# Block-local attention: one resident copy of the value bands, their block sums taken from it, keys in quarters, the score scale moved into the mask addition

## What is computed

```python
k_sum = k.reshape(B, H, nb, block, D).max(axis=3)
v_sum = v.reshape(B, H, nb, block, D).mean(axis=3)
scores_l = scale * np.matmul(q, k.transpose(0, 1, 3, 2))      # kept where |i - j| < 16
scores_s = scale * np.einsum('bhsd,bhnd->bhsn', q, k_sum) + np.log(block)
a = softmax(np.concatenate([scores_l_m, scores_s], axis=-1))
out = np.matmul(a, np.concatenate([v, v_sum], axis=2))
```

## Time and profile before

| | us |
|---|---|
| median of 3 runs (lowest, highest) | 466.71 (465.79, 468.4) |
| the profiled execution, by itself | 468.67 |
| its span, first to last instruction | 466.6 |
| PE busy, share of the span | 427.0, 92% |
| DVE, ACT, POOL busy | 242.4, 188.7, 55.3 |

### The profile page before, as it was taken

The page is one execution under the profiler, slowest core; times in us unless marked ns, Lnnn a source line. Parts: engine busy times, 40 slices in busy tenths (PEclk is TensorE's granted clock), DMA queues, the critical chain, the costliest instruction groups (busy, mean ns, idle before and its releaser), DMA issues.

```text
span 466.6 us, 8147 instructions
## 1 busy us (share of the span) xinstructions
PE 427.0 (92%) x2811; PEld 341.2 (73%) x2812; DVE 242.4 (52%) x381; ACT 188.7 (40%) x425; POOL 55.3 (12%) x96
## 2 busy tenths in 40 slices
PE   8589887298999999999999897999999899999997
PEld 3478776156888888888888654888887688888775
DVE  4678895676226362244511316666666745546252
ACT  1857895702336363363522423333333331222010
POOL 3223421111100010000200054000000000000000
PEclk9978999779999999999999899999999999999999
DMA  8988792845911118211103056000000000000012
GB/s 330 317 265 284 274 340 89 323 150 173 396 63 46 45 45 346 81 45 45 46 22 112 25 155 228 1 0 1 1 0 1 0 24 22 22 24 21 26 45 91
DMA packets 12909, 52.77 MB, mean 113 GB/s; under 512 B 1744, under 2 KB 1872, under 8 KB 11344
## 3 DMA queue, kind: packets, MB, share of 16 engines
q1 hardware_dynamic: 7584, 37.44, 21.8%
q0 software_dynamic: 3424, 11.54, 7.7%
q10 hardware_dynamic: 1872, 3.41, 1.9%
HBM read 61.82 MB, written 11.53 MB: 157 GB/s over the span
## 4 chain that ended last, share of the span: by engine, by line
PE 74%; DVE 12%; ACT 5%; DMA 4%; issue 2%; POOL 0%; DVEq 0%; SPq 0%; ACTq 0%; POOLq 0%
PE ps L1107 14%; PE ps L1109 14%; PE ps L1108 14%; PE ps L1220 6%; PE ps L1222 6%; PE ps L1221 6%; PE ps L1010 2%; PE ps L1185 2%; PE ps L1135 2%; ACT p L527 2%; DMA v<-v_win 2%; PE ps L1114 2%; DMA kfull<-k_full 1%; PE ps L985 1%; PE ps L995 1%
## 5 line engine op out<-in xcount | busy, mean ns | idle before, releaser
L1220 PE MATMUL ps<-z_h,mix_h 128*128 128x512 f32 x144 | 56.9, 395 | 0.9 <-DVE z_l L944 0.9
L1222 PE MATMUL ps<-z_h,mix_l 128*128 128x512 f32 x144 | 56.2, 390 | 0.0
L1221 PE MATMUL ps<-z_l,mix_h 128*128 128x512 f32 x144 | 56.1, 390 | 0.0
L1107 PE MATMUL ps<-w_h,hT_h 128*128 128x512 f32 x104 | 42.3, 407 | 1.9 <-DVE hT_l L856 1.9
L1107 PE MATMUL ps<-w_h,xT_h 128*128 128x512 f32 x104 | 41.6, 400 | 1.9 <-DVE xT_l L850 1.9
L1109 PE MATMUL ps<-w_l,hT_h 128*128 128x512 f32 x104 | 41.4, 398 | 0.0
L1108 PE MATMUL ps<-w_h,hT_l 128*128 128x512 f32 x104 | 41.2, 397 | 0.0
L527 ACT ACTIVATE p<-s,bias 128x120 f32<-128x120 f32 x96 | 36.5, 383 | 11.7 <-DVE bias L707 11.5
L856 DVE TENSOR_TENSOR hT_l<-ps,hT_h 128x512 fp32r<-128x512 f32 x26 | 16.7, 685 | 46.3 <-ACT hT_h L594 46.3
L1109 PE MATMUL ps<-w_l,xT_h 128*128 128x512 f32 x104 | 40.6, 390 | 0.0
L1108 PE MATMUL ps<-w_h,xT_l 128*128 128x512 f32 x104 | 40.6, 390 | 0.0
(11 more groups left out here) (174 smaller groups left out, 857.2 us busy)
## 6 DMA issues: line engine op xcount, KB each, us to landing
w_raw<-w SPq DMA_DIRECT2D x16, 2048.0 KB
v<-v_win SPq DMA_DIRECT2D x24, 192.0 KB, 5.0
mix_raw<-mix SPq DMA_DIRECT2D x1, 4608.0 KB, 13.9
ys<-y_sb ACTq DMA_DIRECT2D x13, 256.0 KB, 2.0
kfull<-k_full SPq DMA_DIRECT2D x4, 800.0 KB, 10.8
vfull_sb<-v_full SPq DMA_DIRECT2D x2, 1536.0 KB, 10.9
xd<-x_sb POOLq DMA_DIRECT2D x12, 256.0 KB, 5.1
out<-o SPq DMA_DIRECT2D x12, 256.0 KB, 2.0
```

Source lines behind the costliest of these rows:

```text
L1107: pe.matmul(ps[:, bank, :], a_h[:, k, :], w_h[:, n, :], start=(k == 0), stop=False)
L1220: pe.matmul(ps[:, t, :], w_h, zh, start=(jb == 0 and m == 0), stop=False)
L1221: pe.matmul(ps[:, t, :], w_h, zl, start=False, stop=False)
L1222: mm = pe.matmul(ps[:, t, :], w_l, zh, start=False, stop=(jb == TPB - 1 and m == 1))
```

## The change

- **Values.** `v_sb` holds the bands of all 12 tiles. Six pairs of loads, two tiles each and 96 rows of 2 x 2 KB, fill it with no wait before any of them; the plain values aren't loaded. `value_summary` multiplies the bands (their inner 64 rows a half) by two averaging matrices, 48 matmuls a batch instead of 24, as each pair arrives. POOL first clears the summary rows of the even halves, which lie under these matmuls.
- **Sums into rows.** For tile 0 DVE copies them from PSUM in eight pieces. For the others POOL copies them from `vsum_sb`, two copies a tile, two tiles ahead.
- **Order.** ACT copies both halves of pT of tile 0 between the exps of tile 1, before the value sums. On PE `transpose_x(g-1)` stands ahead of `weigh(g)`. All loads of attention, then routing's constants and the first expert's weights, are issued one after another.
- **Keys** come in four loads a batch, with the maxima in four parts: for the second batch one behind tile 1, two behind tile 2, one behind tile 3. `q` comes in five parts.
- **Scale.** The mask is kept unscaled, and one `scalar_tensor_tensor` multiplies by 1/8 and adds it; the exps have no scale, the negated maximum is their bias, and the bias instruction is gone. The scores lie at 128 columns a head in PSUM.

The core of the diff, with declarations, semaphores and the host's arrays left out:

```diff
-    mask = np.full((P, 3, NK), MASKED * math.sqrt(D), np.float32)
+    mask = np.full((P, 3, NK), MASKED, np.float32)
...
-        mask[:, m][summary] = math.log(BLOCK) * math.sqrt(D)
+        mask[:, m][summary] = math.log(BLOCK)
-    c[p, C_AVG + NB - P // BLOCK + p // BLOCK] = 1.0 / BLOCK
+    for u in range(2):
+        c[NB * (1 - u) + WINDOW + r, C_AVG + u * AVG_W + NB - SB2 + r // BLOCK] = 1.0 / BLOCK
...
+        vsum_sb = nc.alloc_sbuf_tensor_at("vsum_sb", [NB, DM], f32, offset=at[0])
...
-        v_sb = [sb(f"v{s}", [NK, 2, DM]) for s in range(2)]
+        v_sb = sb("v", [NK, NT, 2, DM])
-        bias = [sb(f"bias{s}", [P, H]) for s in range(2)]
-        vsum_sb = sb("vsum_sb", [NB, DM])
...
-        s_ps = ps[:, B_SC:B_SC + 2, 0:PAIRS * NK].rearrange("p a (b k) -> p a b k", k=NK)
+        s_ps = ps[:, B_SC:B_SC + 2, :].rearrange("p a (b k) -> p (a b) k", k=P)[:, :, 0:NK]
...
-        Q_PARTS = (0, 1, 4, TPB, NT)
+        Q_PARTS = (0, 1, 2, 4, TPB, NT)
...
-            def load_v(g, s):
+            def load_v(n):
-                    sp.dma_start(v_sb[s][NB * (1 - u):NB * (1 - u) + WK, u, :], vwin_d[bass.ds(g, 1), u]).then_inc(v_in[s], 16)
+                    sp.dma_start(v_sb[NB * (1 - u):NB * (1 - u) + WK, 2 * n:2 * n + 2, u, :], vwin_d[u, :, 2 * n:2 * n + 2, :]).then_inc(v_in[n], 16)
-                for a in range(2):
-                    pairs = slice(a * PAIRS // 2, (a + 1) * PAIRS // 2)
-                    sp.dma_start(kfull_sb[b][:, pairs, :], kfull_d[b, :, pairs, :]).then_inc(kfull_in[b][a], 16)
+                for a in range(PAIRS):
+                    sp.dma_start(kfull_sb[b][:, a, :], kfull_d[b, :, a, :]).then_inc(kfull_in[b][a], 16)
-            sp.dma_start(vfull_sb[:, :, :], vfull_d[0]).then_inc(vfull_in, 16)
-            for g in range(2):
-                load_v(g, g)
+            for n in range(TPB // 2):
+                load_v(n)
-            for g in range(2, NT):
-                sp.wait_ge(av_ready, g - 1)
-                load_v(g, g % 2)
-                if g == 2:
-                    load_q(3)
-                if g == 3:
-                    sp.wait_ge(vsum_ready, 1)
-                    sp.dma_start(vfull_sb[:, :, :], vfull_d[1]).then_inc(vfull_in, 16)
-                    sp.dma_start(const[:, C_UT:C_END], const_d[:, C_UT:C_END]).then_inc(rconst_in, 16)
-                if g == NT - 7:
-                    sp.dma_start(w1_raw[:, :, :], w1_d[0]).then_inc(w1_in, 16)
-                if g == NT - 4:
-                    sp.dma_start(w2_raw[:, :, :], w2_d[0]).then_inc(w2_in, 16)
+            load_q(3)
+            for n in range(TPB // 2, NT // 2):
+                load_v(n)
+            load_q(4)
+            sp.dma_start(const[:, C_UT:C_END], const_d[:, C_UT:C_END]).then_inc(rconst_in, 16)
+            sp.dma_start(w1_raw[:, :, :], w1_d[0]).then_inc(w1_in, 16)
+            sp.dma_start(w2_raw[:, :, :], w2_d[0]).then_inc(w2_in, 16)
...
-            pool.memset(zero[:, :], 0.0).then_inc(zeroed, 1)
+            def clear_rows(b):
+                pool.memset(v_sb[0:NB, b * TPB:(b + 1) * TPB, 0, :], 0.0).then_inc(v_clear, 1)
+            clear_rows(0)
...
+                    pairs = slice(a * PAIRS // 2, (a + 1) * PAIRS // 2)
-                        pool.wait_ge(kfull_in[b][a], 16)
-                    pairs = slice(a * PAIRS // 2, (a + 1) * PAIRS // 2)
+                        pool.wait_ge(kfull_in[b][pairs.start], 16)
+                        pool.wait_ge(kfull_in[b][pairs.start + 1], 16)
-                pool.wait_ge(kmax_done, 2 * (b + 1))
+                pool.wait_ge(kmax_done, PAIRS * (b + 1))
...
-            def value_rows(b, s, windows):
-                pool.wait_ge(vsum_out, b + 1)
-                if b:
-                    pool.wait_ge(av_ready, TPB - 1 + s)
+            clear_rows(1)
+            pool.memset(zero[:, :], 0.0).then_inc(zeroed, 1)
+            def value_rows(g, windows):
+                pool.wait_ge(vsum_out, g // TPB + 1)
-                pool.tensor_copy(v_sb[s][0:NB, 0, :], vsum_sb[:, :]).then_inc(rows_set, 1)
-                pool.wait_ge(rows_set, 2 * b + s + 1)
-                pool.tensor_copy(v_sb[s][WK:WK + NB, 1, :], vsum_sb[:, :]).then_inc(vsum_set[s], 1)
-                pool.wait_ge(vsum_set[s], b + 1)
-            for s in range(2):
-                value_rows(0, s, 4)
+                pool.tensor_copy(v_sb[0:NB, g, 0, :], vsum_sb[:, :]).then_inc(rows_even, 1)
+                pool.wait_ge(rows_even, g)
+                pool.tensor_copy(v_sb[WK:WK + NB, g, 1, :], vsum_sb[:, :]).then_inc(rows_set, 1)
+                pool.wait_ge(rows_set, g)
+            pool.wait_ge(v_clear, 2)
+            pool.wait_ge(zeroed, 1)
+            value_rows(1, 4)
-                if TPB - 2 <= g < TPB:
-                    value_rows(1, g % 2, g + 4)
+                if g + 2 < NT:
+                    value_rows(g + 2, min(g + 4, NT))
...
-                if b:
-                    act.wait_ge(vsum_set[1], b)
+                if b == 0:
+                    act.wait_ge(rows_first, 1)
+                else:
+                    act.wait_ge(rows_set, TPB - 1)
-                    act.wait_ge(bias_ready, g + 1)
-                    e = act.activation(p_sb[s][:, n // PAIRS, n % PAIRS, :], s_sb[s][:, n // PAIRS, n % PAIRS, :], ACT.Exp,
-                                       bias=bias[s][:, n:n + 1], scale=1.0 / math.sqrt(D), accum_out=rsum[s][:, n:n + 1])
+                    e = act.activation(p_sb[s][:, n // PAIRS, n % PAIRS, :], s_sb[s][:, n, :], ACT.Exp,
+                                       bias=nmax[s][:, n:n + 1], accum_out=rsum[s][:, n:n + 1])
-            def pT_copy(g):
+            def pT_copy(g, u=0):
-                act.activation(pT[:, 0, :, :], ps[0:NK, B_PT, :].rearrange("p (a k) -> p a k", k=P), ACT.Copy)\
-                   .then_inc(pT_even, 1)
+                act.activation(pT[:, u, :, :], ps[0:NK, B_PT + u, :].rearrange("p (a k) -> p a k", k=P), ACT.Copy)\
+                   .then_inc(pT_odd if u else pT_even, 1)
...
-            for s in range(2):
-                exps(s, s, range(H), first=True)
+            exps(0, 0, range(H), first=True)
+            exps(1, 1, range(0, H // 2), first=True)
+            for u in range(2):
+                pT_copy(0, u)
+            exps(1, 1, range(H // 2, H), first=True)
             vsum_copy(0)
-            pT_copy(0)
...
-            def key_summary(b, halves=range(2)):
-                for a in halves:
-                    half = slice(a * PAIRS // 2, (a + 1) * PAIRS // 2)
+            def key_summary(b, pairs):
+                for a in pairs:
-                    dve.tensor_reduce(out=kmax[:, b * PAIRS + half.start:b * PAIRS + half.stop, :],
-                                      in_=kfull_sb[b][:, half, WINDOW:WINDOW + S].rearrange("p a (n k) -> p a n k", k=BLOCK),
+                    dve.tensor_reduce(out=kmax[:, b * PAIRS + a, :],
+                                      in_=kfull_sb[b][:, a, WINDOW:WINDOW + S].rearrange("p (n k) -> p n k", k=BLOCK),
...
-                dve.tensor_tensor(s_sb[s][:, :, :, :], s_ps, masks[:, edge.get(g % TPB, 1), :].unsqueeze(1).unsqueeze(1).broadcast_to([P, 2, PAIRS, NK]),
-                                  ALU.add).then_inc(scores_taken, 1)
+                dve.scalar_tensor_tensor(s_sb[s][:, :, :], s_ps, 1.0 / math.sqrt(D),
+                                         masks[:, edge.get(g % TPB, 1), :].unsqueeze(1).broadcast_to([P, H, NK]),
+                                         ALU.mult, ALU.add).then_inc(scores_taken, 1)
-                dve.tensor_reduce(out=nmax[s][:, :], in_=s_sb[s][:, :, :, :].rearrange("p a b k -> p (a b) k"),
+                dve.tensor_reduce(out=nmax[s][:, :], in_=s_sb[s][:, :, :],
-                dve.tensor_scalar(bias[s][:, :], nmax[s][:, :], 1.0 / math.sqrt(D), None, ALU.mult).then_inc(bias_ready, 1)
...
-                pT_copy(g)
+                if g:
+                    pT_copy(g)
-            key_summary(0)
+            key_summary(0, range(PAIRS))
             dve.wait_ge(const_in, 16)
             for g in range(2):
                 scores(g, g, first=True)
+            dve.wait_ge(vsum_ready, 1)
+            for u in range(2):
+                for c in range(KD):
+                    e = dve.tensor_copy(v_sb[WK * u:WK * u + NB, 0, u, c * P:(c + 1) * P], ps[CG * c:CG * c + NB, B_VSUM, 0:P])
+            e.then_inc(rows_first, 1)
-                if 1 <= g < 3:
-                    key_summary(1, [g - 1])
+                key_summary(1, {1: [0], 2: [1, 2], 3: [3]}.get(g, []))
...
-                pe.wait_ge(vfull_in, 16 * (b + 1))
+                pe.wait_ge(v_clear, b + 1)
-                    at = C_AVG + NB - P // BLOCK * (j + 1)
-                    for c in range(KD):
-                        mm = pe.matmul(ps[CG * c:CG * c + NB, B_VSUM, 0:P], const[:, at:at + NB], vfull_sb[:, j, c * P:(c + 1) * P],
-                                       start=(j == 0), stop=(j == TPB - 1))
+                    g = b * TPB + j
```

(37 more changed lines are left out.)

28 lines of the change are left out of this document (14 added, 14 removed).

## The result

The changed kernel is slower: a median of 470.4 us (467.43 to 472.69, 20 runs) against 466.97 us of the kernel before on the same chip (464.88 to 469.77, 20 runs). The ratio is 1.0064, its 95% interval 1.0045 to 1.0082, which is 2.1 to 3.8 us. The profiled execution took 468.67 us, with a span of 466.8. So the two traces show where attention changed, but not the whole of the 3.4 us between the medians.

What follows compares the result with a forecast made beforehand. Attention was taken to be bound by handovers, a ring set by ACT at 4.57 us a tile. The terms -0.6 - 4.2 - 0.8 + 1.4 = -4.2 us gave 462.5 us against a median of 466.71, range 457.5 to 467.5.

Steps and rivals of the forecast that it cites:

- Term 1: Start up to weigh(4): 44.9 against 45.47, so -0.6 us, with the second summary's extra 1.45 us included.
- the clock: PE at half clock from the last third of the first summary to scores(2): +1.4 us, of 0 to +2.1.
- The rate: DMA moves the bands at 248 GB/s, so the first sums' bands end at 18.0 and land at 19.3 us.
- What costs nothing: POOL's copies and memsets, SP's loads, keys and queries stay covered; data term 0 to +2, down to -3.6 at 413.
- Rival A: PE at half clock at the start (+2.1) and during the second summary (+2.9): 466.1 us, chance 0.22.
- Rival B: Bands move as fast as other loads, land 3.6 us earlier, and the clock holds: 457.5 us, chance 0.12.
- Rival C: Summary matmuls with 120 and 96 rows don't overlap; 48 take 5.2 us, not 2.9: 471.5 us, chance 0.08.
- Term 2: Steady tiles, weigh(4) to weigh(11): 29.1 us against 33.3, so -4.2 us.
- The ring: Steady tiles: a loop of exps, transpose_p to scores, add and max, pT over two tiles, 8.6 us, 4.3 a tile.
- The first step: weigh(4) to weigh(5), in the steady tiles: 4.3 us instead of 5.70.
- Term 3: Tail behind weigh(11): about 4.5 us against 5.35, as tile 10's share is done earlier: -0.8 us.
- port rule: Loads of bands: 96 partitions would move at about 310 GB/s, three quarters of 413; the time about 459.2 us.

Runs made afterwards that it cites:

- e2: The changed kernel with two and three warm matmuls ahead of PE's second and third waits for bands; ratio 1.0034 to the kernel before.
- e13: The changed kernel with the first expert's weights behind weigh(6) and warm matmuls filling PE's waits in the first summary; ratio 0.9985 to the kernel before.
- e4: The changed kernel with the first expert's two weight loads held behind a wait for weigh(6); ratio 0.9981 to the kernel before.
- e3: The changed kernel with bands laid out over 128 rows, zero rows under the sums, no POOL clearing; ratio 0.9960 to the kernel before.
- e7: The changed kernel with bands over 128 rows and the first expert's weights behind weigh(6); ratio 0.9945 to the kernel before.
- e9: The changed kernel with plain values for the first summary, 128-row bands, first expert's weights behind weigh(6), queries of tiles 4 and 5 earlier; ratio 0.9886.
- e12: The kernel before with transpose_x ahead of weigh, scale in the mask add, and the first expert's weights in eight pieces behind tiles 4 to 11; ratio 0.9928.
- e15: The kernel before with order and scale edits and the first expert's weights in eight pieces, run again on another occasion; ratio 0.9920.
- e8: The changed kernel with weigh put back ahead of transpose_x on PE; ratio 1.0092 to the kernel before.
- e1: The kernel before with only transpose_x ahead of weigh and the scale in the mask add; ratio 0.9987 to the kernel before.
- e11: The kernel before with order and scale edits and both first-expert weight loads behind the last tile's values; ratio 1.0036 to the kernel before.

## Why the prediction was wrong, point by point

**Term 1, the start, forecast -0.6 and +1.4 for the clock; it was +5.84** at weigh(4). The rate was right (248 taken, 241 to 253 measured). The bands landed at 20.3, not 19.3: +1.0. Of that 0.5 is an estimate from the bytes: by 8.5 us DMA had moved 2.30 MB and not 2.44. The rest isn't placed. DVE's eight copies took 2.39 for 2.25. The clock cost 0.84 in the last third and 0.93 of waiting for scores(2), 1.8 for the 1.4 taken, inside my 0 to 2.1; e2 and e13 measure 1.1 to 1.6 net. From DVE's first add to weigh(3) it was 15.33 for 14.97. So weigh(3) stood at 41.42 where 39.4 was forecast with the clock.

The larger part lies behind it. **From weigh(3) to weigh(4) I had 6.9 us and it took 9.89.** The step that failed stands under "What costs nothing": "SP's loads are issued ahead of all use", a term put at nothing. I looked at who waits for each load, and not at what a queue that runs without a pause does to others. Three pairs of kernels differ only in the line that holds back the two weight loads, with them in flight and then without: after and e4 9.89 and 7.06, e2 and e13 11.22 and 7.53, e3 and e7 8.91 and 7.08. It is 1.8 to 3.7 us each time, and it has two parts.

- Breaks on PE: 1.0 of the 2.8 us of the first pair, 2.2 of the 3.7 of the second, none in the third. By all that the traces show they are waits of PE for its own instructions, which come as DMA packets, later with the weights in flight. The last section has the rows.
- Half clock in the second summary and beside it: 1.8, 1.5 and 1.8 us. The summary alone took 4.42 us in the changed kernel and 2.77 in e4 (42.62 to 45.39). All three kernels with the weights in flight had it, and none of their partners. Yet it isn't shown to be the weights' doing: e9 had half clock in the same summary before its weights were issued, and e12 and e15, one and the same kernel, were granted 0.50 and 1.00 from 39.9 to 43.2 us.

**Rival A** (half clock at the start and in the second summary, 466.1 us) named the right two places: 1.8 us for its 2.1 at the start, and 4.42 - 2.9 = 1.5 for its 2.9 in the summary. It lacked the late landing and the breaks. **Rival B** fell with the row of 241; e3 shows what it would have needed. (Its 3.6 us is 3.8 by its own terms, 2.36/0.248 - 2.36/0.413.) **Rival C**, the slower one, was wrong: 96 matmul records take 2.84 us at full clock, in the groups of 120 and 96 rows too. That its 471.5 us is the nearest of my numbers to the 470.4 measured is luck: the kernel is slower for another reason than the one I gave.

**Term 2, forecast -4.2, measured -3.21** (30.11 for 33.32). The ring was right: 8.67 us for two tiles against 8.6, five tiles 21.43 against 21.5. The first step took 5.07 instead of 4.3, with a break of 0.56 in it, and the last 3.61 instead of 3.3. With the weights later (e4) the first step took 4.27. The ring needed both the order and the other edits (e8), and nothing of the bands (e1).

**Term 3, forecast -0.8, measured -0.84**. **The scale** added nothing, as forecast: the add still takes 1.16 us. No `weigh` waited for v_win, and the POOL copies were hidden.

The sum in the trace: 5.84 - 3.21 - 0.84 = +1.79 us. The runs say 2.1 to 3.8. The two profiled executions don't settle the difference: behind attention, in the same code, they took 382.35 us before and 380.8 after, which gives most of the 1.79 back. The breaks at this place ran from 0.8 to 2.5 us between traces, so the executions with the larger ones may make the median; that is an argument and not shown.

On the port rule (the Trainium skill, "SBUF — State Buffer", section Door 1: The DMA port swizzle: a transfer's rate follows how many ports its partitions reach): e3 agrees with its direction, since 128 rows move at 385 to 393 GB/s. The page counts the ports that are reached, and the three quarters is my estimate from its table of ports. The size isn't that of the estimate: 96 rows had 0.64 of that (248 by 389), and not 0.75.

## What to carry to other kernels

A load without a wait before it isn't free when nothing waits for it: see what runs on the other engines while it moves, and put a large one where that is slack, or cut it up so that it fits between the transfers that someone needs soon. A steady rhythm and its transfers must be mended together; the ring alone (e1) gave 0.1%, the place of the weights with it (e12) 0.7 to 0.8%. When a load is moved later, follow the queue to the next small transfer behind it (e11). And a long list of small matmuls needs transfers of its own, for its instructions: where it is densest, keep the DMA engines from being full.
